# Swapping the operands of one out-product in a fused convolution and two-layer kernel

## The reference

```python
# x: (2, 4096, 192), K = 7 taps, softmax over the taps of each of 8 heads, causal
out = np.einsum('hk,bskhg->bshg', softmax(weight), x_unfolded)      # -> (8192, 192)
# layer 1: w_in (192, 2048), w_out (2048, 192)
h = x @ w_in;  g = h * np.clip(h + 3.0, 0.0, 6.0) / 6.0;  x = g @ w_out
# layer 2: w_in (192, 2048), w_out (2048, 192), a (4), b (2)
h = x @ w_in
P = a[0] + a[1]*h + a[2]*h**2 + a[3]*h**3
Q = 1.0 + abs(b[0])*abs(h) + abs(b[1])*h**2
return (P / (Q + 1e-06)) @ w_out                                   # (8192, 192), float32
```

## Time and profile before

| what | value |
|---|---|
| median of 3 runs | 1202.07 us (1201.59 to 1202.16) |
| the profiled execution's own time | 1204.0 us |
| its span, first to last instruction | 1201.9 us |
| granted TensorE clock, mean | 0.998 |
| TensorE (PE) busy, instructions | 99%, 5145 matmuls |
| weight loads (PEld) busy | 80%, 5145 |
| VectorE (DVE) / ScalarE (ACT) / GpSimd (POOL) busy | 97% / 89% / 89% |
| read and written in HBM | 14.60 MB, 6.29 MB |

### The profile page before, as it was taken

How to read it: one execution, slowest core, us unless ns; L and a number is a source line. 1 busy time by engine, 2 the same in 40 slices (tenths; PEclk the granted TensorE clock), 3 DMA queues, 4 the chain that set the end, 5 groups by cost and what they waited for, 6 DMA issues and landing times. The chain is left out here.

```text
span 1201.9 us, 17842 instructions
## 1 busy us (share of the span) xinstructions
PE 1186.5 (99%) x5145; PEld 963.2 (80%) x5145; DVE 1160.7 (97%) x1784; ACT 1065.5 (89%) x1980; POOL 1072.9 (89%) x829
## 2 busy tenths in 40 slices
PE   8999999999999999999999999999999999999998
PEld 6778888888888888888888888888888888888754
DVE  7999999999999999999999999999999999998898
ACT  7888899898998988989998899889999899888886
POOL 5989989898998989999898998999989899898874
PEclk9999999999999999999999999999999999999999
DMA  4400000000000000010000000000000000000010
GB/s 147 152 2 10 1 23 1 23 10 23 1 1 24 9 23 1 1 32 1 22 1 15 17 2 23 1 23 10 1 23 1 23 1 1 14 1 14 1 44 13
DMA packets 11313, 22.02 MB, mean 18 GB/s; under 512 B 1744, under 2 KB 3152, under 8 KB 11216
## 3 DMA queue, kind: packets, MB, share of 16 engines
q1 hardware_dynamic: 10928, 20.89, 5.9%
q10 hardware_dynamic: 288, 0.01, 0.0%
HBM read 14.60 MB, written 6.29 MB: 17 GB/s over the span
## 5 line engine op out<-in xcount | busy, mean ns | idle before, releaser
L525 POOL TENSOR_TENSOR den<-den,sqr 128x512 f32<-128x512 f32 x246 | 360.7, 1466 | 92.3 <-ACT den L499 91.1
L599 POOL TENSOR_TENSOR g_lo<-g,g_hi 128x512 fp32r<-128x512 f32 x246 | 319.4, 1298 | 7.9 <-ACT g_hi L605 7.9
L492 POOL TENSOR_TENSOR g_lo<-r,g_hi 128x512 fp32r<-128x512 f32 x235 | 309.9, 1319 | 1.7 <-ACT g_hi L605 1.3
L605 ACT ACTIVATE g_hi<-g 128x512 fp32r<-128x512 f32 x246 | 155.9, 634 | 54.9 <-PE y1b_acc L385 47.1
L529 ACT ACTIVATE rsq<-den 128x512 f32<-128x512 f32 x246 | 155.0, 630 | 45.6 <-POOL den L525 42.7
L519 DVE SCALAR_TENSOR_TENSOR num<-h,monic,num 128x512 f32<-128x512 f32 x246 | 184.6, 751 | 8.2
L513 DVE SCALAR_TENSOR_TENSOR num<-h,monic,sqr 128x512 f32<-128x512 f32 x246 | 183.2, 745 | 0.0
L552 DVE SCALAR_TENSOR_TENSOR h<-num,monic,h 128x512 f32<-128x512 f32 x238 | 178.3, 749 | 0.2
L478 DVE SCALAR_TENSOR_TENSOR r<-r,h 128x512 f32<-128x512 f32 x235 | 160.4, 683 | 14.2 <-ACT r L471 13.4
L545 DVE SCALAR_TENSOR_TENSOR den<-den,h 128x512 f32<-128x512 f32 x238 | 161.9, 680 | 1.0 <-ACT h L541 0.9
L574 DVE SCALAR_TENSOR_TENSOR g<-den,h 128x512 f32<-128x512 f32 x238 | 161.1, 677 | 0.2
(11 more groups left out here) (182 smaller groups left out, 2886.8 us busy)
## 6 DMA issues: line engine op xcount, KB each, us to landing
stage_w<-w_pack SPq DMA_DIRECT2D x16, 448.0 KB, 3.4
raw_a<-x_a SPq DMA_DIRECT2D x16, 259.0 KB, 3.2
out<-y_a SPq DMA_DIRECT2D x16, 256.0 KB, 2.0
out<-y_b SPq DMA_DIRECT2D x16, 128.0 KB, 2.3
raw_b<-x_b SPq DMA_DIRECT2D x14, 129.5 KB, 2.7
r<-w_pack SPq DMA_DIRECT2D x4, 96.0 KB, 2.0
raw_b<-x_b SPq DMA_DIRECT2D x4, 65.5 KB, 4.6
y_a<-w_pack SPq DMA_DIRECT2D x2, 96.0 KB, 2.3
```

Of the source, the lines that this page charges most:

```text
L492: eng.tensor_tensor(g1_lo[t % 2][:, :], gated(t)[:, :], f32(g1_hi[t % 2][:, :]), ALU.subtract).then_inc(S["g1lo"], 1)
L525: eng.tensor_tensor(den_of(t), den_of(t), sqr_of(t), ALU.add).then_inc(S["den_sum"], 1)
L599: eng.tensor_tensor(g2_lo[t % 2][:, :], g2[t % 2][:, :], f32(g2_hi[t % 2][:, :]), ALU.subtract).then_inc(S["g2lo"], 1)
L605: return eng.activation(dst, src, ACT.Copy)
```

## The change

It has two parts.

1. *Layer 2's out-product has its operands swapped.* Now 128 tokens of g are the stationary operand, and the 192 columns of the weights stream. The result is by token: 128 tokens on partitions, 192 features along the free dimension. A block of 512 tokens is four such groups of 128; two of them share a bank (`y2_acc`, 2 x 192 columns of 512). For each group there are three matmuls (g_hi x w_hi, g_hi x w_lo, g_lo x w_hi), twelve per tile. The hi pass has two matmuls in turn with the same stationary slice, the lo pass one per group. The stored weights of a tile are now 192 columns of hi and 192 of lo (L857 and on). The unsplit tiles take four matmuls, one per group, against 192 whole columns. `y2a_out` copies the first two groups, `y2b_out` (in place of `y2b_move` and `y2b_sum`) the other two: both on ScalarE, in the last block `y2b_out` on VectorE. The kernel's output is (batch, token, 192), each store writing two runs of 192 numbers per partition. Six of the nine unsplit weight tiles go to spare columns of the staging buffers, and SP loads them before the stores of block 13; the other three are loaded before those of block 14.
2. *The numerator's set-up* stands in steps 12 to 18 in place of 5 to 11, at the end of VectorE's list. The plans name `y2b_out` where they had `y2b_move`, and the waits of `num2` and `g_neg` are in another order. Layer 1's out-product stays as it was.

```diff
 START = {
-    "vector": [("monic_side", 5), ("monic_safe", 6), ("monic_inverse", 7), ("monic_c2", 8), ("gate1", 0), ("monic_ratio", 9),
-             ("monic_c01", 10), ("monic_scale", 11), ("conv_b1", AHEAD, (2, 2, 2, 3, 5, 6, 7), 1), ("g1lo", 1),
+    "vector": [("gate1", 0), ("conv_b1", AHEAD, (2, 2, 2, 3, 5, 6, 7), 1), ("g1lo", 1),
...
 BEGIN = {
-             ("x2b_res", SUM1, 0), ("g1lo", 1), ("x2b_lo", SUM1, 0), ("conv_a", AHEAD, (6, 4, 4, 16, 4, 5))],
+             ("x2b_res", SUM1, 0), ("g1lo", 1), ("x2b_lo", SUM1, 0), ("conv_a", AHEAD, (6, 4, 4, 16, 4, 5)),
+             ("monic_side", 12), ("monic_safe", 13), ("monic_inverse", 14), ("monic_c2", 15), ("monic_ratio", 16),
+             ("monic_c01", 17), ("monic_scale", 18)],
...
 MIDDLE = {
-    "scalar": [("y2b_move", SUM2, 0), ("y2a_out", SUM2, 0), ("cs_b_hi", AHEAD, 13, 0),
+    "scalar": [("y2b_out", SUM2, 0), ("y2a_out", SUM2, 0), ("cs_b_hi", AHEAD, 13, 0),
-             ("cs_b_lo", AHEAD, 15, 0), ("y2b_sum", SUM2, 0), ("g_neg", 2), ("gate1", 0), ("newton", 1),
+             ("cs_b_lo", AHEAD, 15, 0), ("g_neg", 2), ("gate1", 0), ("newton", 1),
...
-        WO = DA + P + DA
+        D = DA + DB
+        WO = 2 * D
...
+        y2_acc = [bank(f"y2_acc{i}") for i in range(2)]
...
-        spent = [r1[0], r1[1], y_a[0], raw_a[1], x2b_rest]
-        w_full = {t: spent[i // 2][:, i % 2 * (DA + DB):(i % 2 + 1) * (DA + DB)] for i, t in enumerate(full)}
+        spent = [st[:, BLK:BLK + 2 * D] for st in stage_w] + [r1[0], r1[1], y1_a, raw_a[1], x2b_rest]
+        w_full = {t: spent[i // 2][:, i % 2 * D:(i % 2 + 1) * D] for i, t in enumerate(full)}
+        in_stage = full[:2 * W_STAGES]
...
+        def tokens(i):
+            return slice(i * P, (i + 1) * P)
+
+        def y2_of(i):
+            return y2_acc[i // 2][:, i % 2 * D:(i % 2 + 1) * D]
...
+        def out_product2_hi(eng, t):
+            k, f = divmod(t, NF)
+            w, g_hi = wout[1][:, f * WO:(f + 1) * WO], g2_hi[t % 2]
+            for i in range(BLK // P):
+                y, g = y2_of(i), g_hi[:, tokens(i)]
+                if f == 0 and i % 2 == 0:
+                    after(eng, S[("y2a_out", "y2b_out")[i // 2]], k)
+                eng.matmul(y, g, w[:, 0:D], start=f == 0 and i % 2 == 0, stop=False, skip_group_check=True)
+                eng.matmul(y, g, w[:, D:WO], start=False, stop=False, skip_group_check=True)
+
+        def out_product2_lo(eng, t, groups):
+            f = t % NF
+            for i in groups:
+                ins = eng.matmul(y2_of(i), g2_lo[t % 2][:, tokens(i)], wout[1][:, f * WO:f * WO + D],
+                                 start=False, stop=f == NF - 1, skip_group_check=True)
+            return ins
...
         def pe_out2(eng, t):
...
-                eng.matmul(ya_acc[1][:, :], w[:, 0:DA], g, start=False, stop=False)
-                eng.matmul(yb_acc[1][0:DB, :], w[:, DA:DA + DB], g, start=False, stop=False) \
-                    .then_inc(S["n2_done"], 1)
+                for i in range(BLK // P):
+                    ins = eng.matmul(y2_of(i), g2[t % 2][:, tokens(i)], w_full[t], start=False, stop=False,
+                                     skip_group_check=True)
+                ins.then_inc(S["n2_done"], 1)
...
-                out_product(eng, 1, t, g2_hi[t % 2], g2_lo[t % 2], ("y2a_out", "y2b_sum")) \
-                    .then_inc(S["n2_done"], 1)
+                out_product2_hi(eng, t)
+                out_product2_lo(eng, t, range(4)).then_inc(S["n2_done"], 1)
...
+            out_product2_hi(eng, t)
             eng.wait_ge(S["g2lo"], splits(t))
+            out_product2_lo(eng, t, range(2)).then_inc(S["n2a_done"], 1)
+            out_product2_lo(eng, t, range(2, 4)).then_inc(S["n2_done"], 1)
...
+            eng.activation(y2_half(0), y2_acc[0][:, 0:2 * D], ACT.Copy, scale=minus_scale).then_inc(S["y2a_out"], 1)
+
+        def y2b_out(eng, k):
+            if (k == NB - 1) != (eng is nc.vector):
+                return
+            eng.wait_ge(S["n2_done"], (k + 1) * NF)
+            after(eng, d_out_b, 16 * k)
...
+            scaled(eng, y2_half(1), y2_acc[1][:, 0:2 * D], minus_scale).then_inc(S["y2b_out"], 1)
...
         def store_y(eng, k):
+            if k == NB - 3:
+                load_w_full(eng, in_stage, d_w_stage, ("w_in_done", 2 * n_chunks), ("w_out_done", 2 * n_chunks))
...
+            for half, name, landed in ((0, "y2a_out", d_out_a), (1, "y2b_out", d_out_b)):
+                rows = out[k % 2, bass.ds(k // 2 * BLK + half * HALF, HALF), :]
+                eng.wait_ge(S[name], k + 1)
+                eng.dma_start(rows.rearrange("(g p) d -> p g d", p=P),
+                              y2_half(half).rearrange("p (g d) -> p g d", d=D)).then_inc(landed, 16)
```

More of the change, by code:

```diff
@@ L104 @@
              ("x2b_hi", SUM1, -10), ("sq2", 0), ("rec2", 1), ("y2a_out", SUM2, 2), ("g2hi", 2),
-             ("y2b_move", SUM2, 3)],
-    "vector": [("num2", 1), ("y2b_sum", SUM2, 0), ("num1", 1), ("g_neg", 2), ("x2b_res", SUM1, -3), ("g2lo", 6),
+             ("y2b_out", SUM2, 3)],
+    "vector": [("num2", 1), ("num1", 1), ("g_neg", 2), ("x2b_res", SUM1, -3), ("g2lo", 6),
              ("x2b_lo", SUM1, -2), ("newton", 1), ("g_first", 1)],
@@ L139, in build_program @@
     XW, HW = BLK + K - 1, HALF + K - 1
-    assert n_batch == 2 and n_layers == 2 and DA + DB == out.shape[0] and DB * 2 == P
+    assert n_batch == 2 and n_layers == 2 and DA + DB == out.shape[2] and DB * 2 == P
     assert SPARE == NT - NF
@@ L210, in build_program @@
         conv_a, conv_b = sb("conv_a", BLK), sb("conv_b", BLK)
-        y_a = [sb(f"y{l}_a", BLK) for l in range(2)]
-        y2_b = sb("y2_b", BLK, F32, DB)
+        y1_a = sb("y1_a", BLK)
+        y2 = sb("y2", BLK // P * D)
         x2b_rest = sb("x2b_rest", BLK)
@@ L254, in build_program @@
         h_banks = [bank(f"h_{i}") for i in range(H_BANKS)]
-        ya_acc = [bank(f"y{l}a_acc") for l in range(2)]
-        yb_acc = [bank(f"y{l}b_acc") for l in range(2)]
-        yb_last = h_banks[bank2[NT - H_BANKS]][0:DB, :]
+        y1a_acc, y1b_acc = bank("y1a_acc"), bank("y1b_acc")
+        y2_acc = [bank(f"y2_acc{i}") for i in range(2)]
         def h1_of(t):
@@ L368, in in_product, with out_product1 @@
             return mm
-        def out_product(eng, l, t, g_hi, g_lo, left):
+        def out_product1(eng, t, g_hi, g_lo):
             k, f = divmod(t, NF)
-            c = f * WO
-            w = wout[l]
+            w = wout[0][:, f * WO:(f + 1) * WO]
             first, last = f == 0, f == NF - 1
-            a_hi, b_hl, a_lo = w[:, c:c + DA], w[:, c + DA:c + DA + P], w[:, c + DA + P:c + WO]
+            a_hi, b_hl, a_lo = w[:, 0:DA], w[:, DA:DA + P], w[:, DA + P:WO]
             if first:
[L378 to L381, removed]
+                after(eng, S["y1a_out"], k)
+            eng.matmul(y1a_acc[:, :], a_hi, g_hi[:, :], start=first, stop=False)
+            eng.matmul(y1a_acc[:, :], a_lo, g_hi[:, :], start=False, stop=False)
+            eng.matmul(y1a_acc[:, :], a_hi, g_lo[:, :], start=False, stop=last)
@@ L382, in out_product @@
             if first:
-                after(eng, S[left[1]], k)
-            eng.matmul(yb_acc[l][:, :], b_hl, g_hi[:, :], start=first, stop=False)
-            return eng.matmul(yb_acc[l][:, :], b_hl, g_lo[:, :], start=False, stop=last)
+                after(eng, S["x2b_lo"], k)
+            eng.matmul(y1b_acc[:, :], b_hl, g_hi[:, :], start=first, stop=False)
+            return eng.matmul(y1b_acc[:, :], b_hl, g_lo[:, :], start=False, stop=last)
+        def tokens(i):
+            return slice(i * P, (i + 1) * P)
@@ L439, in pe_out2 @@
                 eng.wait_ge(S["g2lo"], splits(t))
-                out_product(eng, 1, t, g2_hi[t % 2], g2_lo[t % 2], ("y2a_out", "y2b_sum")) \
-                    .then_inc(S["n2_done"], 1)
+                out_product2_hi(eng, t)
+                out_product2_lo(eng, t, range(4)).then_inc(S["n2_done"], 1)
                 spare_products(eng, t)
                 return
[L447 to L451, removed]
             eng.wait_ge(S["g2hi"], splits(t))
-            eng.matmul(ya_acc[1][:, :], a_hi, g_hi[:, :], start=False, stop=False)
-            eng.matmul(ya_acc[1][:, :], a_lo, g_hi[:, :], start=False, stop=False)
-            for i, w in enumerate(b):
-                eng.matmul(yb, w, g_hi[:, :], start=last and i == 0, stop=False)
+            out_product2_hi(eng, t)
             eng.wait_ge(S["g2lo"], splits(t))
-            eng.matmul(ya_acc[1][:, :], a_hi, g_lo[:, :], start=False, stop=last).then_inc(S["n2a_done"], 1)
-            for i, w in enumerate(b):
-                ins = eng.matmul(yb, w, g_lo[:, :], start=False, stop=i == len(b) - 1)
-            ins.then_inc(S["n2_done"], 1)
+            out_product2_lo(eng, t, range(2)).then_inc(S["n2a_done"], 1)
+            out_product2_lo(eng, t, range(2, 4)).then_inc(S["n2_done"], 1)
         def gated(t):
-            return [ya_acc[1], yb_acc[1]][t % 2] if t < EARLY else r1[t % 2]
```

(1 more changed line is left out.)

95 lines of the change are left out of this document (41 added, 54 removed).

## The result

| | before | changed |
|---|---|---|
| median | 1202.12 us (4 runs, 1201.59 to 1202.17) | 1255.85 us (4 runs, 1255.16 to 1257.33) |
| ratio | | 1.0446, 95% interval 1.0433 to 1.046 |
| profiled execution, its time and span | 1204.0, 1201.9 us | 1256.28, 1254.5 us |
| one step of both layers | 4.53 us, 20 matmuls | 4.75 us, 27 matmuls |

The change costs 53.7 us. The forecast was 1273, in a range of 1222 to 1292: the sign and the engine were right, the cost was put 17 us too high. One of the four executions of the run in "Fewer loads, the same columns" took 1461.6 us at a mean granted clock of 0.753, and its number there leaves that one out.

The account below looks back on a forecast made before the run. TensorE's instruction pace was taken to bound the kernel from 80 to 1137 us. Out-product +71.9, set-up +0.3 and end -0.6 gave +71.6, rounded to +71 and added to the median 1202.07: 1273 us, range 1222 to 1292.

Parts of the forecast that it names:

- the stretch and its bound: From 80 to 1137 us, TensorE's pace of taking instructions sets the time, 0.227 us per matmul.
- loads aren't left out, and a load occupies about 107 ns: Layer 2's out-product: loads rise from 5 to 12 per tile, each 128-column load holding the loading path for 107 ns.
- load plus the same 13: Each new out-product slot takes 0.120 us, a load and 13 ns: +0.306 us per tile, +71.9 us over 235 tiles.
- the lower end: Lower bound for a new out-product slot: 0.110 us, the spacing of loads alone, +43.7 us.
- the rival of 0.14: The load alone sets the out-product's slot, 0.110 us: 1245 us; chance 0.14.
- the set-up's move: Numerator's set-up at steps 12 to 18, some 44 to 58 us: +0.3 us, bounds 0 and +1.5.
- the end: After 1137 us: split tiles mostly absorbed, the last chain shorter; together -0.6 us, bounds -1.5 and +2.
- The stream as the only price: The 12 new out-product matmuls go at their stream, 93 ns per slot, -3.4 us: 1198 us; chance 0.12.
- A shared load: The hi pass's pair of matmuls shares one load, 1.227 us per tile, +22 us: 1224 us; chance 0.06.
- Four passes for narrow streams: The out-product's narrow matmuls lose the fast path, 333 ns each, +673 us: 1875 us; chance 0.05.

Follow-up runs that it names:

- Fewer loads, the same columns: The changed kernel with the hi pass's two matmuls made one of 384 columns, loads falling from 12 to 8 per tile: 1217.7 us, ratio to before 1.0134.

## Why the prediction was right, and where it was wrong

**Right: the stretch and its bound.** TensorE alone sets 80 to 1190 us, in both kernels; it has no wait there, and 235 tiles carry the cost. No other engine was the bound, though VectorE, busy 1039 of the 1110 us, is not far from it.

**Right: loads aren't left out, and a load occupies about 107 ns.** 6908 loads for 6908 matmuls; loads of 128 columns follow each other at 0.112 us. The swap was to pay below 0.0945 us per slot, and only the runs with smaller loads reached that (0.088, 0.060). With 0.088 the time was that of the kernel before and no better: what the slots gain, the 512-column matmuls behind them lose (last section).

**Wrong in size: "load plus the same 13".** The prediction took 0.120 us per slot from the warm-up's 256 columns, where stream and load are both 107 ns, and put the 13 ns on the longer of the two. The runs give 0.112 where the load alone binds (192 and 128 columns) and 0.119 with 256 ((601.23 - 599.80) / 12 in that run's timeline). So the excess belongs to the stream or to the two being equally long, and a load that is the longer has 4 or 5 ns on it. Per tile 12 x 0.008 = 0.1 us, over 235 tiles 23 us: 71.9 becomes 49, and the steps measured give 51. The row for the right value, 0.11 between two loads, was in hand as the lower end and as the rival of 0.14. It was the nearer one in what binds, although the 256-column row was the nearer in shape; and 1255.85 lies between that rival's 1245 and the forecast, nearer the rival. What lifts it over 1245 is mainly 0.112 in place of 0.110 (6 us) and the start (3 us). (The lower end of the forecast's own range adds up to 1264 by its terms, not 1262.)

**Wrong in size: the set-up's move.** +0.3, bounds 0 and +1.5, were given. The runs show +3.3 (changed kernel against the one with the set-up back) and about +3.0 (alone on the kernel before, executions with the same early stretch compared). The prediction let only the last operation count; all but the last stood ahead of the end of VectorE's chain to x1b_hl, and three of them took 0.62 to 1.01 us, each until a GpSimd instruction ended. The 2.5 idle us of VectorE in 40 to 60 us were no cover, since most of them lie before 50 us and behind 58.3 us: from 50 to 58.3 us it is busy 7.94 of 8.30.

```profile
50.00:58.30 8.30, 7.35 (x32) 5.45 (x30) 7.94 (x12) 7.46 (x15) 8.10 (x10) 1.00 0.68 219
```

The lower clock that followed the wait was not priced at all. With the slot put 23 us too high and the set-up 3 us too low, the errors cancel in small part.

**Right: the end.** From the last product of layer 1 to the end the kernel before needs 1201.9 - 1135.7 = 66.2 us, the changed one 1254.5 - 1188.8 = 65.7: -0.5 where -0.6 was forecast. The ten split tiles there were absorbed; the wait of the out-product for g_lo grew from 1.5 to 5.4 us, which is idle time of TensorE in a stretch that VectorE sets. That the sum fits is in part luck: a whole-precision tile became 0.8 us shorter (last section), where 0.3 at most was forecast.

The sum with what was measured: 51 + 3.3 - 0.5 = 53.8, against 53.7. Its terms come from profiled executions and from medians, so the last digit is no proof.

**The rivals.** The stream as the only price (1198) falls: with 128 columns less stream changes no slot. With it falls, for these fp32r operands, the line of the Trainium skill, "TensorE: Matmul & The Clock Gate", section "Back-to-back issue gap", of about 81 ns for a load and matmul of 128 columns: here that shape takes 0.11. The same page's section "LDWEIGHTS (loading the stationary operand)" gives columns / 1.2 GHz, 107 ns for 128, and the trace agrees nearly, with 0.112 from load to load. A shared load (1224) falls by the count. Four passes for narrow streams (1875) fall: 192 columns go at 0.088 and 128 at 0.060 once the load is small.

## What to carry to other kernels

Count stationary loads, not only streamed columns: before operands are swapped, work out for each new matmul the longer of its stream and the next operand's load (here 0.112 us for 128 fp32r columns, so with 192 streamed columns the load sets the slot, and with 256 no longer alone). Where two prices could hold, take the row in which the same resource binds rather than the one whose shape looks nearest, and keep the other as the end of the range. When small operations are moved, an engine's share below 100% does not make the new place free: look at what stands behind them in its list, at what runs beside them (here a 128 x 1 operation on VectorE took up to 1.24 us and ended with a GpSimd instruction), and at the clock that TensorE is granted after a wait.

## What the runs showed of the hardware that was not expected

- The excess of a slot over its stream isn't constant: slots of 0.060 us for 128 columns (53 ns of stream), 0.088 for 192 (80), 0.119 for 256 with a load as long (107), 0.175 for 384 (160), 0.227 for 512 (213). The first two were measured with loads of 64 columns.
- Behind a group of narrow matmuls, 512-column ones take up to 0.232 us in place of 0.227 for the next nine, at a granted clock of 1.00. The cause is open. The table has the means over all full steps from 90 to 1110 us: the narrow group, the first 512-column slot behind it (which can hold the wait for its own load), and the 14 others.

| stationary, streamed columns | narrow slots, us | first wide slot | 14 others |
|---|---|---|---|
| the kernel before | | 0.227 | 3.17 |
| 128, 192 (changed) | 1.32 | 0.253 | 3.18 |
| 128, 384 and 192 | 1.13 (8 slots) | 0.251 | 3.21 |
| 64, 192 | 1.08 | 0.253 | 3.19 |
| 128, 128 | 1.29 | 0.289 | 3.22 |
| 128, 256 | 1.43 | 0.234 | 3.19 |

- Three operations on 128 x 1 with two operands, on VectorE, ended 0.02 us behind the GpSimd instruction that ran beside them, after up to 1.01 us; with one operand they took 0.14 to 0.16.
- The wait of 2.1 us in the changed kernel was followed by more than 6 us at 1.2 GHz. In the six other runs whose longest wait for x1b_hl is 2.1 to 2.3 us, the stretch was about half as long (with 64 tokens stationary the granted clock was 0.96 in 58 to 60 us, 0.50 in 60 to 62 and 0.69 in 62 to 64); a wait of 1.3 us, with others just before, was followed by a short stretch, too.
- Whole-precision matmuls gained from the swap. A tile of four of them, with its eight records, starts at 1236.08 in the changed kernel, and the second matmul of the in-product behind it at 1237.61: 1.53 us. Before, the same distance was 2.29 us: 1.96 to the first in-product matmul and 0.33 from there to the second. Nine of 256 tiles are too few to matter.

```profile
1236.08 1.46 PE L463 MATMUL y_acc<-r,g 128*128 128x192 f32 x8
...
1237.61 0.39 PE L371 MATMUL h<-x1a_hi,win_lo 128*128 128x512 f32 x1
```
